# The two first tiles of the most frequent expert, routed from half of the tokens, prepared during attention

## The chip, the cores and the metric

One core of one Trainium2 chip runs the whole program. The metric is device time in microseconds of an execution. The engines are called as the profile calls them: PE (TensorE matmul; PEld its weight loads), DVE (VectorE), ACT (ScalarE), POOL (GpSimd), SP (SyncE, here a queue of DMA issues).

## What is computed

Three layers in float32, one after the other:

```
scores = q @ k^T / 8                     # 4 batches, 8 heads, 576 rows, 64 columns
keep scores >= row max - tau (0.02), softmax, @ v         -> x [2304, 512]
logits = x @ w_gate + modality_bias[modality_id]          # 8 experts
e = argmax(logits); gate = softmax(logits)[e]
out[row] = gate * (relu(x[row] @ w1[e]) @ w2[e])          # w1 512x1024, w2 1024x512
h = out @ w_in; g = h * sigmoid(1.702 h); result = g @ w_out   # w_in 512x2048
```

The modality bias (spread 0.5) dwarfs what x adds to the logits, so a row's expert is nearly its modality's. With the reference's inputs 2043 rows go to expert 1 and 261 to expert 4; of the 1152 rows of the first two batches, 1011 go to expert 1.

## The kernel before

The five engines run programs of their own that are tied by semaphores; each engine's order is the order in which its program is written.

**Attention.** Heads are handled in 16 pairs (one head of two batches), two pairs to a "quad"; pairs 0 to 7 belong to the first two batches. A pair has nine units of 128 query rows (`U = 9`), and a quad 18 steps. In step `i` PE transposes the probabilities of a unit five steps back and the q and k of the next pair (L1191, L1205), makes a unit's scores (L1225), and in steps u = 1 and 5 of a pair the product with v of the pair before (L1239), in u = 3 and 7 its turn to rows (`turn`, L1256 to L1264). DVE scales the scores with their row minimum (L760) and masks the unit of two steps earlier (L715); ACT exponentiates (L1038) and copies the transposed blocks out of PSUM (L1001, L1012); POOL makes the threshold (`thresh`, L626), splits the next pair's q and k in high and low parts (`split`, L576, L578) and swaps halves of k. `over_quads` writes quad 0 out, loops over quads 1 to 6, and writes quads 7 and 8 out (quad 8 has the last values and no scores).

Matrix products are exact to float32 by three passes: a high part in the reduced format, a low part (`x - high`), and high·high + low·high + high·low. Weights are loaded raw, copied to high by ACT (L1105), subtracted to low by DVE (L918).

**Routing.** After the last head DVE runs a chain of small operations, each waiting for the one before (`link`): logits of all 18 row tiles, the expert of each row, gates; PE counts rows per tile and expert (L1306, L1307); DVE works out each row's place in the list sorted by expert and two one-hot matrices (L838 to L844); PE multiplies them to the list of rows `table` (L1313); DVE writes the plan (tiles of 256 rows: `PL_AT` first place, `PL_END` the end of an expert's turn). The list is turned, stored in DRAM (`order_dram`), the gates too.

**Experts.** POOL gathers a tile's rows and gates by indirect DMA (L647, L649): the first from `table`, later ones after loading their indices from `order_dram` (L660). DVE scales, PE transposes (L1323), ACT and DVE split. Then `up` (L1332, 96 matmuls) and `down` (L1345, 96 matmuls). `over_turns` loops over the experts in use; `enter` splits the expert's weights, `body` does a tile and transposes the next one ahead. `tile_x` is a single buffer: the gather of tile t+1 waits for the transposes of tile t. SP loads an expert's eight weight pieces (L521, L527) once the previous expert's have been split. At the end comes the dense layer (L1378, L1395).

The first lines of `over_turns` and of PE's `body`:

```
with eng.Fori(0, turns) as turn:
    first = eng.value_load(plan_i[...PL_END + turn...])
    enter(turn, first)
    with eng.Fori(first, end) as tile:  body(turn, tile)
# PE's body:  up(tile); transpose_x(tile + 1); down(turn, tile)
```

## Time and profile before

| what | us |
|---|---|
| median of 3 runs (1042.2 to 1042.96) | 1042.36 |
| the profiled execution | 1042.66 |
| its span | 1041.0 |
| attention, to PE's last turn | 342.6 |
| from there to the first expert matmul | 40.1 |
| ten expert tiles | 382.8 to 624 |
| dense layer | to the end |

The span is what the profile sees between first and last instruction; 1.66 us lie around it. Busy: PE 976.8 us (94%), DVE 483.3 (46%), ACT 442.2 (42%), POOL 258.1 (25%). An engine that is busy most of the time in one stage can stand idle in the next, so the page's slices and the stretches are read stage by stage. All numbers of a timeline are microseconds from the span's start.

### The profile page before, as it was taken

The page shows a single profiled execution, that of the slowest core. Times are in us where ns is not written, and L with a number is a line of the kernel's source. Part 1 is how long each engine was busy: PE and PEld are TensorE (multiplying, and loading weights), DVE is VectorE, ACT ScalarE, POOL GpSimd, SP SyncE. Part 2 cuts the span into 40 slices and gives each one's busy share as a digit, 9 for nine tenths or more (in the row PEclk, how much of TensorE's full clock was granted, in tenths as well). Part 3 has the DMA queues.
Part 4 walks back from the last instruction along what each step waited for, and adds up shares of the span by engine and source line. Part 5 has one row for each costly group of instructions (what it writes and reads, how often), then busy time and mean ns, then how long its engine had stood idle before and what let it go on. Part 6 is the DMA issues. An engine that isn't in the chain of part 4 may idle for free.

```text
span 1041.0 us, 19901 instructions
## 1 busy us (share of the span) xinstructions
PE 976.8 (94%) x6496; PEld 870.6 (84%) x6497; DVE 483.3 (46%) x1076; ACT 442.2 (42%) x1004; POOL 258.1 (25%) x360
## 2 busy tenths in 40 slices
PE   5999999999998339999999999999999999999994
PEld 5777878778786239999999998989999999999994
DVE  6878778787787642212113335532322223222221
ACT  4777878787786041112113335432222222222221
POOL 5655656556552031112222100010010010100101
PEclk9999999999999659999999999999999999999998
DMA  3232222222211084111111443210000000000000
GB/s 81 49 64 63 51 63 58 54 64 63 60 31 24 12 278 146 40 40 40 50 50 41 149 144 112 61 52 11 31 30 0 30 30 30 31 0 0 31 1 31
DMA packets 103422, 57.18 MB, mean 55 GB/s; under 512 B 84917, under 2 KB 93659, under 8 KB 103387
## 3 DMA queue, kind: packets, MB, share of 16 engines
q1 hardware_dynamic: 92072, 40.15, 14.4%
q0 software_dynamic: 4224, 10.51, 3.2%
q10 hardware_dynamic: 7091, 6.08, 1.8%
q8 instruction: 18, 0.29, 0.1%
q14 instruction: 17, 0.14, 0.0%
HBM read 41.49 MB, written 15.22 MB: 54 GB/s over the span
## 4 chain that ended last, share of the span: by engine, by line
PE 89%; DVE 3%; issue 2%; POOL 1%; ACT 1%; DMA 1%; ACTq 0%; SPq 0%; POOLq 0%; DVEq 0%
PE s_ps L1395 19%; PE s_ps L1378 13%; PE s_ps L1332 11%; PE o_ps L1239 8%; PE pt_ps L1191 8%; PE s_ps L1225 8%; PE pt_ps L1378 6%; PE misc L1345 6%; PE o_ps L1345 6%; PE pt_ps L1205 3%; PE pt_ps L1323 1%; PE misc L1264 1%; PE misc L1256 1%; DVE probs L715 0%; DMA qk<-in_k_dram 0%
## 5 line engine op out<-in xcount | busy, mean ns | idle before, releaser
L978 DVE TENSOR_TENSOR g<-s_ps,sig 128x384 f32<-128x384 f32 x96 | 53.5, 558 | 279.1 <-ACT sig L1162 279.1
L1162 ACT ACTIVATE sig<-s_ps 128x384 f32<-128x384 f32 x96 | 47.2, 492 | 273.5 <-PE s_ps L1395 273.5
L760 DVE TENSOR_SCALAR_CACHE_REDUCE scores<-s_ps,taus 128x576 f32<-128x576 f32 x144 | 117.8, 818 | 61.9 <-PE s_ps L1225 39.8
L715 DVE SCALAR_TENSOR_TENSOR probs<-scores,thresh,probs 128x576 f32<-128x576 f32 x144 | 130.8, 909 | 0.0
L1191 PE MATMUL pt_ps<-ident,probs 128*128 128x128 f32 x720 | 126.7, 277 | 4.0 <-ACT pT L1001 2.7
L1395 PE MATMUL s_ps<-yT_high,w_in_high 128*128 (+1 forms) x384 | 129.5, 337 | 0.3 <-issue 0.2
L1395 PE MATMUL s_ps<-yT_high,w_in_low 128*128 (+1 forms) x384 | 129.5, 337 | 0.0
L1395 PE MATMUL s_ps<-yT_low,w_in_high 128*128 (+1 forms) x384 | 128.9, 336 | 0.0
L669 POOL DMA_INDIRECT out_dram<-out_sb,table x18 | 18.9, 1049 | 419.6 <-ACT out_sb L1137 416.0
L1038 ACT ACTIVATE probs<-scores,row_low 128x576 f32<-128x576 f32 x144 | 115.5, 802 | 10.9 <-DVE scores L760 9.2
L1191 PEld LDWEIGHTS pt_ps<-ident,probs 128*128 128x128 f32 x720 | 84.0, 140 | 26.6 <-issue 19.5
L626 POOL TENSOR_TENSOR thresh<-row_low,taus 128x1 f32<-128x1 f32 x144 | 74.0, 514 | 121.9 <-DVE scores L760 114.3
L1225 PE MATMUL s_ps<-qkT 128*128 128x288 f32 x320 | 101.7, 335 | 2.5 <-DVE k_swap L709 0.6
L1332 PE MATMUL s_ps<-xT_high,w_high 128*128 128x256 f32 x320 | 91.6, 286 | 8.8 <-DVE w_low L918 8.5
L1239 PE MATMUL o_ps<-pT,vv 128*64 128x320 f32 x640 | 93.2, 437 | 0.8 <-ACT pT L1001 0.8
L1332 PE MATMUL s_ps<-xT_low,w_high 128*128 128x256 f32 x320 | 91.2, 285 | 0.0
L1332 PE MATMUL s_ps<-xT_high,w_low 128*128 128x256 f32 x320 | 91.2, 285 | 0.0
L1225 PE MATMUL s_ps<-k_swap,qkT 128*128 128x288 f32 x320 | 89.2, 295 | 0.0
L1001 ACT COPY pT<-pt_ps 128x512 f32<-128x512 f32 x144 | 85.3, 592 | 8.8 <-PE pt_ps L1191 6.1
L908 DVE SCALAR_TENSOR_TENSOR hT_low<-s_ps,hT_high 128x512 fp32r<-128x512 f32 x40 | 27.6, 691 | 113.8 <-ACT hT_high L1082 113.8
L1395 PEld LDWEIGHTS s_ps<-yT_high,w_in_high 128*128 128x128 f32 x384 | 72.2, 188 | 5.1 <-issue 1.0
L1378 PE MATMUL s_ps<-w_out_high,g_low 128*128 128x512 f32 x192 | 76.2, 397 | 0.0
(209 smaller groups left out, 2205.5 us busy)
## 6 DMA issues: line engine op xcount, KB each, us to landing
w_raw<-in_moe_w_dram SPq DMA_DIRECT2D x16, 512.0 KB, 4.6
yT_dram<-tile_yT ACTq DMA_DIRECT2D x11, 512.0 KB, 2.9
x_dram<-xs SPq DMA_DIRECT2D x32, 128.0 KB, 2.0
w_in_raw<-in_moe_w_in_dram SPq DMA_DIRECT2D x4, 1024.0 KB, 6.2
w_out_raw<-in_moe_w_out_dram SPq DMA_DIRECT2D x16, 256.0 KB, 2.6
qk<-in_k_dram SPq DMA_DIRECT2D x30, 128.0 KB, 2.4
next_yT<-yT_dram SPq DMA_DIRECT2D x5, 768.0 KB, 4.5
qk<-in_q_dram SPq DMA_DIRECT2D x16, 128.0 KB, 2.2
```

Source lines behind the costliest of these rows:

```text
L626: pool.tensor_tensor(thresh[:, j, u:u + 1], row_low[:, j, u:u + 1], taus[:, 4:5], ALU.add).then_inc(thresh_ready, 1)
L715: dve.scalar_tensor_tensor(out=probs[:, i % PROB_SLOTS, 0:SEQ], in0=scores[:, i % SCORE_SLOTS], scalar=thresh[:, j, u:u + 1], in1=probs[:, ...
L760: dve.tensor_scalar(scores[:, i % SCORE_SLOTS].rearrange("p (c n) -> p c n", c=2), s_ps[i % 2][:, :, 0:HALF], taus[:, 3:4], None, ALU.mult ...
L1001: act.copy(pT[:, 0:TAIL, v * P:(v + 1) * P], pt_ps[:, 0:TAIL]).then_inc(keys_copied, 1)
L1038: act.activation(probs[:, k % PROB_SLOTS, 0:SEQ], scores[:, k % SCORE_SLOTS], ACT.Exp, bias=row_low[:, k // U, k % U:k % U + 1], scale=-1. ...
L1191: return pe.transpose(pt_ps[:, block], probs[:, k % PROB_SLOTS, block * P:(block + 1) * P], ident[:])
L1225: mm = pe.matmul(s_ps[i % 2][:, c, 0:HALF], qkT[j][:, 0, q_tile * P:(q_tile + 1) * P], keys[:, first:first + HALF], start=(at == 0), stop= ...
L1239: mm = pe.matmul(o_ps[lo:lo + DH, 0:UP], vv[j][:, side, block], pT[:, block, at:at + UP], start=(block == 0), stop=(block == TPB - 1))
L1332: mm = pe.matmul(hT_ps[f // 2][:, f % 2 * T:(f % 2 + 1) * T], w_part[:, a, f * P:(f + 1) * P], x_part[:, a], start=(a == 0 and part == 0), ...
L1345: mm = pe.matmul(yT_ps[d // 2][:, d % 2 * T:(d % 2 + 1) * T], w_part[:, f, d * P:(d + 1) * P], h_part[:, f], start=(f == 0 and part == 0), ...
L1378: mm = pe.matmul(mlp_y_ps[i], g_part[:, f % GT, at], w_part[:, f, :], start=(f == 0 and part == 0), stop=(f == FB2 - 1 and part == 2))
L1395: mm = pe.matmul(mlp_h_ps[f % 2], w_part[:, a, f * P:(f + 1) * P], y_part[:, bass.ds(c % 2 * DB + a, 1)].rearrange("p a b -> p (a b)"), st ...
```

## The change

- After pair 7 the first two batches are complete. `half_logits(0)`, `half_choice(0)`, `half_gates(0)` route their 1152 rows during quads 4 and 5; PE counts them in two small matmuls. `early_expert` picks the most frequent expert and limits its early rows to 512; `early_members` to `early_one_hots` make the list of its first 512 rows (two tiles), which PE writes in quad 6 (nine small matmuls).
- SP stores the first half's gates, loads the expert's w1 in quad 6 and w2 in quad 7. ACT and DVE split w1 in quad 7, one piece in each of four steps. POOL gathers tile 0 in steps 2 and 7 of quad 7. Part of `up(0)` stands between attention's last steps in quad 8, w2's split beside it.
- The full routing then runs beside the rest of `up(0)`, `down(0)`, `up(1)`. Experts are renumbered so that the early one is 0 and its early rows are the list's first 512; the plan counts tiles from 2 on (`EARLY`). Turn 0 is written out; `over_turns` runs from turn 1, which is the same expert again, its weights loaded and split a second time.
- Buffers are laid out anew so that the weights don't cover what attention still uses (w1_high over `xs0`, w2_raw over `qk`, and so on). Quads 4 to 7 are written out on all engines, SP's whole loop too. Gates are stored without being transposed, as single columns.

The core of the diff, first what holds for all engines:

```diff
+    EARLY = 2
+    EARLY_SLOTS = EARLY * T // P
...
-            with eng.Fori(1, QUADS - 1) as quad:
+            with eng.Fori(1, QPB) as quad:
                 step(quad)
-            for quad in range(QUADS - 1, last):
+            for quad in range(QPB, last):
                 step(quad)
```

On SP:

```diff
+            def early_part(quad, j):
+                if (quad, j) == (QUADS - 2, 0):
...
+                    store_gates(0)
+                if (quad, j) == (QUADS - 2, 1):
+                    sp.wait_ge(first_expert_ready, 1)
+                    load_w1(sp.value_load(first_expert_i[0:1], min_val=0, max_val=E - 1), 0)
+                if (quad, j) == (QUADS - 1, 1):
+                    sp.wait_ge(turned, UNITS)
+                    sp.wait_ge(order_stored, 16)
+                    load_w2(sp.value_load(first_expert_i[0:1], min_val=0, max_val=E - 1), 0)
...
+            store_gates(1)
+            sp.wait_ge(order_rows_ready, 1)
+            sp.dma_start(order_dram[0:N].rearrange("(t p) -> t p", p=P), order_rows[:]).then_inc(order_stored, 16)
             sp.wait_ge(plan_ready, 1)
```

On POOL:

```diff
+                    if isinstance(quad, int) and quad == QUADS - 1 and i in (2, 7):
+                        pool.wait_ge(x_stored[0], PAIRS // 2 * 4 * 16)
+                        pool.wait_ge(gate_stored, 4 * 16)
+                        pool.wait_ge(early_list_ready, 1)
+                        gather(early_list, 0, (2, 7).index(i), N // 2)
...
+                    if isinstance(quad, int) and quad == QUADS - 1 and i in (6, 10):
+                        pool.wait_ge(tile_x_loaded, (6, 10).index(i) * 32 + 32)
...
+            for tile in range(1, EARLY):
+                pool.wait_ge(xT_written, tile * 2)
                 for i in range(2):
+                    gather(early_list, tile * 2, i, N // 2)
```

On DVE:

```diff
+            def early_part(quad, i):
+                if (quad, i) == (QPB, 2):
+                    bias_of_rows()
+                if (quad, i) == (QPB, 11):
+                    half_logits(0)
+                if (quad, i) == (QPB, 14):
+                    half_choice(0)
+                    early_hot()
+                if (quad, i) == (QPB + 1, 0):
+                    half_gates(0)
+                if (quad, i) == (QPB + 1, 2):
+                    early_expert()
+                if (quad, i) == (QPB + 1, 5):
+                    early_members()
+                if (quad, i) == (QPB + 1, 9):
+                    early_places()
+                if (quad, i) == (QPB + 1, 12):
+                    early_split()
+                if (quad, i) == (QPB + 1, 15):
+                    early_one_hots()
+                if (quad, i) == (QPB + 2, 4):
+                    early_list_part()
+                if quad == QUADS - 1 and i in (2, 6, 11, 15):
+                    a = (2, 6, 11, 15).index(i)
+                    split_w_low(w1_low, w1_raw, w1_high, w1_high_ready, w1_low_ready, a, a)
+                if (quad, i) == (QUADS - 1, 13):
+                    scale_x(0)
+                if quad == QUADS and i in (6, 7):
+                    split_w_low(w2_low, w2_raw, w2_high, w2_high_ready, w2_low_ready, i - 6, i - 6)
+                if (quad, i) == (QUADS, 2):
+                    xT_low_part(0, first_xT_ps)
```

On ACT:

```diff
+            def early_part(quad, i):
+                if (quad, i) == (QPB, 16):
+                    half_expos(0)
+                if quad == QUADS - 1 and i in (1, 5, 10, 14):
...
+                    split_w_high(w1_high, w1_raw, w1_loaded, w1_high_ready, 0, (1, 5, 10, 14).index(i))
+                if (quad, i) == (QUADS, 2):
+                    xT_high_part(0, first_xT_ps)
+                if quad == QUADS and i in (6, 7):
...
+                        split_w_high(w2_high, w2_raw, w2_loaded, w2_high_ready, 0, a)
```

On PE (the first piece is in `transpose`):

```diff
+                if extra in ("ranks", "totals"):
+                    pe.wait_ge(hot_ready, 1)
+                    pe.matmul(extra_ps[:, 0:U * E], (before if extra == "ranks" else ones)[:],
+                              hot[:, 0:U].rearrange("p t e -> p (t e)"), start=True, stop=True)
+                if extra == "list":
...
+            def early_part(quad, i):
+                if (quad, i) == (QUADS, 0):
+                    pe.wait_ge(low_ready, UNITS - 1)
+                    transpose_x(0, first_xT_ps)
+                if (quad, i) == (QUADS, 4):
...
+                if quad == QUADS and i in (4, 5, 6):
+                    up_block(FIRST_UP[i - 4])
...
+            for f in FIRST_UP[3:6]:
+                up_block(f)
...
+            for f in FIRST_UP[6:]:
+                up_block(f)
...
+            transpose_x(1)
+            pe.wait_ge(w2_low_ready, DB)
+            for d in range(2):
+                down_block(0, d)
+            pe.wait_ge(hT_low_ready, 4)
             pe.wait_ge(one_hot_ready, 2)
             for n in range(RT):
                 mm = pe.matmul(table_ps, row_hot[:, n], slot_tok[:, n], start=(n == 0), stop=(n == RT - 1))
             mm.then_inc(table_written, 1)
+            pe.wait_ge(ranks_read, 1)
+            for d in range(2, DB):
+                down_block(0, d)
             pe.wait_ge(order_ready, 1)
             pe.transpose(order_ps, order_sq[:], ident[:]).then_inc(order_turned, 1)
...
+            pe.wait_ge(table_ready, 1)
+            pe.wait_ge(xT_low_ready, 4)
+            for f in range(FB1):
+                if f == 2:
+                    pe.wait_ge(order_rows_ready, 1)
+                up_block(f)
+            transpose_x(2)
+            down(1)
             pe.wait_ge(plan_ready, 1)
-            transpose_x(0)
             over_turns(pe, enter, body)
```

(An `up_block` is 12 matmuls, a `down_block` 24.)

**Where rows move on POOL.** POOL's program in steps 1 to 7 of quad 7, attention's pair 14, before (in square brackets the semaphores waited for; `qk_parts` is what PE transposes in step 5):

```order
L586 COPY k_swap_51<-qkT_49 64x576 [waits turned_copied,thresh_ready]
L588 COPY k_swap_51<-qkT_49 64x576 [waits k_swapped]
L626 TENSOR_TENSOR thresh<-row_low,taus 128x1 [waits probs_ready,low_ready,k_swapped]
L576 CAST qk_parts<-qk 128x8x64 [waits turned,qk_b_loaded]
L578 TENSOR_TENSOR qk_parts<-qk,qk_parts 128x8x64 [waits parts_ready]
L626 TENSOR_TENSOR thresh<-row_low,taus 128x1 [waits probs_ready,low_ready] x4
L586 COPY k_swap_52<-qkT_50 64x576 [waits turned_copied,thresh_ready]
L588 COPY k_swap_52<-qkT_50 64x576 [waits k_swapped]
```

and with the change:

```order
L654 COPY k_swap_55<-qkT_53 64x576 [waits turned_copied,thresh_ready]
L656 COPY k_swap_55<-qkT_53 64x576 [waits k_swapped]
L687 DMA tile_x<-x_dram,early_list 128x512 [waits gate_stored,early_list_ready,x_stored0,k_swapped]
L689 DMA tile_gate<-gate_dram,early_list 128x1
L705 TENSOR_TENSOR thresh<-row_low,taus 128x1 [waits probs_ready,low_ready]
L644 CAST qk_parts<-qk 128x8x64 [waits turned,qk_b_loaded]
L646 TENSOR_TENSOR qk_parts<-qk,qk_parts 128x8x64 [waits parts_ready]
L705 TENSOR_TENSOR thresh<-row_low,taus 128x1 [waits probs_ready,low_ready] x4
L654 COPY k_swap_56<-qkT_54 64x576 [waits turned_copied,thresh_ready,tile_x_loaded]
L656 COPY k_swap_56<-qkT_54 64x576 [waits k_swapped]
L687 DMA tile_x<-x_dram,early_list 128x512 [waits gate_stored,early_list_ready,x_stored0,k_swapped]
L689 DMA tile_gate<-gate_dram,early_list 128x1
```

The two indirect DMAs of tile 0's first half stand ahead of step 2's threshold and of the split, and a second two ahead of step 7's threshold.

**Where rows move on DVE.** DVE's program with the change, from the one-hot `hot` of all rows (after the last head) to the scaling of tile 2; between the pieces stand the small operations of routing that are also there before:

```order
L1015 TENSOR_TENSOR hot<-expert_less,choice 128x144 [waits route]
...
L921 TENSOR_TENSOR w_low<-w_raw,w_high 128x1024 [waits w2_high_ready] x2
L927 TENSOR_SCALAR tile_x<-tile_x,tile_gate 128x512 [waits tile_x_loaded] x2
L1022 COPY in_tile<-misc 128x144 [waits tiles_counted]
...
L940 SCALAR_TENSOR_TENSOR hT_low<-s_ps,hT_high 128x512 [waits hT_high_ready,route]
L940 SCALAR_TENSOR_TENSOR hT_low<-s_ps,hT_high 128x512 [waits hT_high_ready] x3
L1034 TENSOR_TENSOR place_e<-place_e,rows_first 128x144 [waits ranks_read]
...
L1048 TENSOR_TENSOR slot_hot<-place_slot,iota_row 128x324 [waits x_stored1,split_ready]
L1052 TENSOR_TENSOR slot_tok<-slot_hot,token_id 128x324 [waits split_ready]
L1054 TENSOR_TENSOR row_hot<-place_row,iota_row 128x2304
L933 TENSOR_TENSOR xT_low<-pt_ps,xT_high 128x512 [waits xT_high_ready] x2
...
L1109 CAST order_rows<-s_ps 18x128 [waits order_turned]
L940 SCALAR_TENSOR_TENSOR hT_low<-s_ps,hT_high 128x512 [waits hT_high_ready] x3
L927 TENSOR_SCALAR tile_x<-tile_x,tile_gate 128x512 [waits tile_x_loaded] x2
```

The chain of routing, which stood alone, now has the low parts of w2 and of tiles 0 and 1 in between, and `order_rows` ahead of tile 1's `hT_low`.

## Rows read from the trace of the kernel before

**Rows 1.** Stretches: us, busy time of each engine (instructions), granted clock, DMA share, GB/s

```profile
182.00:208.00 26.00, 25.89 (x202) 20.47 (x199) 20.48 (x53) 19.93 (x50) 15.28 (x22) 1.00 0.25 55
312.00:338.00 26.00, 23.34 (x169) 16.48 (x167) 19.73 (x56) 16.79 (x38) 6.58 (x11) 1.00 0.10 24
```

**Rows 2.** PE timeline: start us, us, line, operation, out<-in [idle before <-releaser]

```profile
341.92 0.70 PE L1264 MATMUL misc<-turn_and_gate,oT 128*128 128x144 f32 x4
...
347.76 0.84 PE L1306 MATMUL misc<-hot,before 128*128 128x144 f32 x2 [5.13 <-DVE hot L807]
...
356.38 4.01 PE L1313 MATMUL o_ps<-slot_tok,row_hot 128*128 128x18 f32 x18 [7.08 <-DVE row_hot L844]
...
372.32 1.94 PE L1323 MATMUL pt_ps<-ident,tile_x 128*128 128x128 f32 x8 [9.12 <-DVE tile_x L895]
...
382.78 0.57 PE L1332 MATMUL s_ps<-xT_high,w_high 128*128 128x256 f32 x1 [8.51 <-DVE w_low L918]
```

**Rows 3.** DVE timeline, routing and the first gathered tile

```profile
343.23 2.21 DVE L800 TENSOR_REDUCE logits<-xs 128x144 f32<-128x1152 f32 x1
...
353.77 2.55 DVE L844 TENSOR_TENSOR row_hot<-place_row,iota_row 128x2304 fp32r<-128x2304 f32 x1
...
362.41 0.18 DVE L884 CAST plan_i<-plan 1x64 int32<-1x64 f32 x1
...
371.30 0.88 DVE L895 TENSOR_SCALAR tile_x<-tile_x,tile_gate 128x512 f32<-128x512 f32 x2 [7.77 <-DMA tile_gate<-gate_dram,table]
```

**Rows 4.** Chain that ended last, expert tiles: start us, us, what

```profile
382.78 13.35 PE s_ps L1332 x96
...
408.50 11.52 PE s_ps L1332 x96
...
432.40 11.52 PE s_ps L1332 x96
...
576.11 11.77 PE s_ps L1332 x96
```

**Rows 5.** Stretches in the gap and after it; PEclk is the column after POOL

```profile
343.00:346.00 3.00, 0.00 (x0) 0.00 (x0) 2.90 (x4) 0.00 (x0) 0.00 (x0) 0.90 0.26 56
386.00:387.00 1.00, 1.00 (x9) 1.00 (x9) 1.00 (x2) 0.41 (x1) 0.05 (x1) 0.82 0.62 226
```

**Rows 6.** Groups by form: busy us, mean ns of one | idle before

```profile
L918 DVE TENSOR_TENSOR w_low<-w_raw,w_high 128x1024 fp32r<-128x1024 f32 x16 | 18.4, 1221 | 8.5 <-ACT w_high L1105 8.5
...
L908 DVE SCALAR_TENSOR_TENSOR hT_low<-s_ps,hT_high 128x512 fp32r<-128x512 f32 x40 | 27.6, 691 | 113.8 <-ACT hT_high L1082 113.8
```

**Rows 7.** DVE and PE timelines, around bias_of_rows in pair 15

```profile
315.76 0.67 DVE L735 TENSOR_SCALAR mod_zero<-mod_one 128x18 f32<-128x18 f32 x1
...
317.98 0.81 DVE L760 TENSOR_SCALAR_CACHE_REDUCE scores<-s_ps,taus 128x576 f32<-128x576 f32 x1
...
318.95 0.37 PE L1225 MATMUL s_ps<-qkT 128*128 128x288 f32 x1 [0.17 <-DVE scores L760]
```

**Rows 8.** POOL and PE timelines, pair 14 of attention

```profile
297.82 0.64 POOL L626 TENSOR_TENSOR thresh<-row_low,taus 128x1 f32<-128x1 f32 x1 [0.66 <-PE pt_ps L1191]
...
299.09 1.29 POOL L578 TENSOR_TENSOR qk_parts<-qk,qk_parts 128x512 fp32r<-128x512 f32 x1
...
302.13 0.19 POOL L626 TENSOR_TENSOR thresh<-row_low,taus 128x1 f32<-128x1 f32 x1 [1.09 <-DVE scores L760]
...
300.81 0.38 PE L1205 MATMUL pt_ps<-ident,qk_parts 128*128 128x128 f32 x2
```

**Rows 9.** POOL timeline, index load and gather of the second tile

```profile
376.18 0.99 POOL L647 DMA_INDIRECT tile_x<-x_dram,tile_index  x1 [3.35 <-DMA tile_index<-order_dram]
...
380.10 1.97 POOL L649 DMA_INDIRECT tile_gate<-gate_dram,tile_index  x1 [0.30 <-issue]
...
385.30 0.75 POOL L660 DMA_DIRECT2D tile_index<-order_dram  x1 [3.23 <-DMA tile_gate<-gate_dram,tile_index]
```

**Rows 10.** SP's issues of an expert's w1: start us, us until all four are issued

```profile
364.50 6.56 SPq L521 DMA_DIRECT2D w_raw<-in_moe_w_dram  x4
```

More of the change, by code:

```diff
@@ L656, in _ @@
             tiles = tiles_of(pool)
-            with pool.Fori(1, tiles + 1) as tile:
-                at = place_of(pool, tile + 1)
+            with pool.Fori(EARLY, tiles + 1) as tile:
+                at = place_of(pool, tile)
                 wait_apart(pool, tile_x_loaded, tile * 64)
@@ L1337, in down @@
-            def down(turn, tile):
-                wait_apart(pe, w2_low_ready, (turn + 1) * DB + 1)
-                wait(pe, tile_yT_copied, tile * 2 + 2)
-                for d in range(DB):
-                    for f in range(FB1):
-                        if d == 0 and f % 2 == 0:
-                            wait(pe, hT_low_ready, tile * 4 + f // 2 + 1)
-                        for part, (w_part, h_part) in enumerate(((w2_high, hT_high), (w2_high, hT_low), (w2_low, hT_high))):
-                            mm = pe.matmul(yT_ps[d // 2][:, d % 2 * T:(d % 2 + 1) * T], w_part[:, f, d * P:(d + 1) * P],
-                                           h_part[:, f], start=(f == 0 and part == 0), stop=(f == FB1 - 1 and part == 2))
-                    if d % 2 == 1:
-                        mm.then_inc(tile_yT_written, 1)
```

620 lines of the change are left out of this document (399 added, 221 removed).

## The prediction

> **What bounds the kernel now.** I read the stretches first, then each engine's timeline where PE is not busy. Through attention PE is the bound: in a stretch of 26 us it is busy 25.89 us, DVE 20.48, ACT 19.93, POOL 15.28; in the stretch that reaches into attention's tail PE has already 2.66 us without work [rows 1]. The PE timeline shows the hole behind it: the last turn of attention starts at 341.92 and ends at 342.6, the first expert matmul starts at 382.78, and between them stand only a few small products, each behind a wait [rows 2]. So 40.1 us pass in which the critical work is DVE's chain of routing (343.23 to 362.6 [rows 3]), the first gather (DVE has tile 0 at 371.30 after 7.77 us of waiting for it [rows 3]) and the split of w1 (8.51 us of waiting on DVE [rows 2]). From then on PE is the bound again: a tile costs 23.9 us (408.50 to 432.40 [rows 4]) and the first one 25.7 (382.78 to 408.50), for the clock had halved: it averages 0.90 from 343 to 346, which puts the fall (from 2.4 to 1.2 GHz) at about 345.4, 2.8 us after PE's last work, and it comes back during 386 to 387, 3.4 us after the first expert matmul [rows 5].
>
> **The change, part by part.** I keep before's times as the clock and add attention's extra length, s, at the end.
>
> *In attention (s).* PE gets two counts of 72 columns: one of 144 columns takes 0.84 us at half clock [rows 2], so half the columns at full clock a quarter, 0.4 us for both, and nine list products, 4.01/18 = 0.22 us each at half clock, 0.11 at full, 1.0 us [rows 2]: 1.4 us on PE, which has no slack. ACT copies these three results between its copies of the transposed blocks: 0 if covered, 3 x 0.18 (a small operation [rows 3]) if not; I take 0.5, since PE waits for those copies each step.
>
> DVE gets some 45 small operations of 0.2 to 0.3 us, a one-hot of half the size of row_hot (1.3 us of 2.55 [rows 3]), four low parts of w1 (4 x 1.22 [rows 6]) and scaling (0.88 [rows 3]): 16 us in quads 4 to 7, which have 160 us and of them 21% idle, 34 us [rows 1]. What an insertion costs PE is shown by one that is there now: bias_of_rows holds DVE from 315.6 to 317.98, 2.4 us, and PE then waits 0.17 us [rows 7]. No inserted piece is longer than 1.7 us, and most stand in steps next to a values product. I take 0.3 us for all; the other end is in the rivals. ACT's four copies of w1 (taken as long as DVE's low parts, 1.22) stand where PE does a values product: nothing. What covers them is that product; without it they would cost 4.9.
>
> POOL gets the first gather pair ahead of step 2's threshold and split in pair 14. In before that threshold starts at 297.82, the split ends at 300.38 and PE takes its result at 300.81: slack 0.43 us [rows 8]. Two indirect DMAs cost 2x + 0.3 us with x between 0.95 and 1.97 (0.99, and 1.97 beside a busy DVE [rows 9]). With x = 1.2, near the many and not the one, PE waits 2.7 - 0.4 = 2.3 us. The second pair (step 7) delays only a threshold that DVE needs some 3 us later: nothing at this x. SP puts w1 and w2 (6.56 us to issue four pieces [rows 10]) ahead of loads of v and q that are issued over 10 us ahead of their use: nothing; were that lead gone, each would cost up to 6.6. That quads 4 to 7 are written out costs nothing I can see: pairs 14 and 15 were already. **s = 1.4 + 0.5 + 0.3 + 2.3 = 4.5 us.**
>
> *End of attention.* Quad 8 takes up eight transposes (0.9) and three blocks of up(0), 12 matmuls x 0.12 = 1.44 each (11.52/96 [rows 4]), 5.2 together, and in exchange fills 2.7 us of waits (2.66 by 338 [rows 1]): PE's last turn ends at 345.1 instead of 342.6.
>
> *Routing beside PE.* PE: five blocks (7.2) and the counts (two of 0.84 at half clock, 0.65 with their start) to 352.95, transposes of tile 1 to 353.8. DVE until then: the second half's logits to hot, 3.5 us (half of 2.21 and eleven small ones), gates 0.65, two low parts of w2 2.2 (their high parts are done at 344), scaling 0.9, and then, before hT_low, six operations of routing, 1.9: at 354.8 it starts hT_low (0.69 each [rows 6]), so PE starts down(0) at 355.55: **1.75 us waited.** Two of its blocks end at 361.3. DVE goes on: four hT_low, eight small operations, the two one-hots and row_hot (2.55) to 362.95: **1.65 us waited.** The table takes 2.0 us at full clock, two more blocks 5.76, the order's transpose 0.25: 370.95. up(1) needs nothing late and ends at 382.5. Both waits are under the 2.8 us after which the clock fell.
>
> *Tile 2 is late next.* DVE reads the turned order after the low part of tile 1 (1.4), 21 plan operations (4.6), and 15 more (3.2): 372.7. Its store (no row shows its landing; a later load's 3.35 us of waiting [rows 9] bounds it above, an issue of 0.3 below, and I take 2.4, nearer the load), POOL's loads of the plan (0.5), the index load (0.75 + 3.35 = 4.1 [rows 9]) and the gather (from 376.18 to 385.30 is 9.1 us [rows 9]; the first one 7.6 to DVE's start at 371.30) follow one another: 388.3 with 8.6 for the gather; scaled at 389.2. **PE waits 6.7 us** (3 to 10, if each link is at its short or long end). The clock falls again, so the eight transposes take 1.94 us [rows 2] and not 0.87, and down(1) starts slow: 11.5 + 0.75. The turn change that follows costs 0.3 us of issue, as between the tiles at 576.11 [rows 4]; the second split of the same expert (eight pieces x 1.22 = 9.8 us on DVE [rows 6]) lies beside down(1) and up(2). up(2) starts at 389.2 + 1.95 + 12.25 + 0.35 = 403.75; in before it starts at 432.40 [rows 4]. That is 28.65 us earlier, less s = 4.5: **24.1 us.** Eight tiles and the dense layer remain as they were. Against the profiled execution, 1042.66 - 24.1 = 1018.5; that execution stands 0.3 us over the median, so I leave 1018.5 as it is. A measurement of this kernel tells 0.2% (2 us) from no change.
>
> **The rivals.**
> - *Tile 2 is nearly in time.* All links short: the stall is 2 us, below 2.8, and the clock stays, which gives back 4.7 + 1.8: 1012. For: at tile 2's gather DVE does little that could slow it. Against: four links must all be at their short end, 7.6 us and less for the gather alone.
> - *Attention doesn't absorb the insertions.* For: DVE's idle is in pieces of 0.2 to 1.2 us, so half of the 16 us may fall on PE: +8, 1026.5. Against: bias_of_rows [rows 7].
> - *POOL's indirect DMAs are held up by DVE.* The same threshold takes 0.64 us or 0.19 [rows 8], depending on what DVE does, and one gather step took 1.97 for 0.99 [rows 9]. If an indirect DMA can run only in DVE's 21% idle [rows 1], x = 1.05/0.21 = 5 us, the two pairs hold PE for (2x - 0.1) + (2x - 2.9) = 4x - 3 = 17 us instead of 2.3: 1033. The Trainium skill's page "SBUF — State Buffer" (SBUF: two separate sides, and the part on the bandwidth-pool intuition) says that DVE and GpSimd share a port pair by an exclusive lock and that descriptors made by GpSimd starve meanwhile, 620 ns becoming 3100. By that factor of five on the 1.0 us here the estimate is the same 17 us and 1033; the trace bears out a factor of two once and none in three others.
> - *Slower than before*: the same mechanism, further. Without any gather stall the change gives 26.4 us; 4x - 3 exceeds that from x = 7.4 us. At 8 us each: 1045. Only steady DVE work with no gap would do it, and attention has gaps.
> - *No early tile gained.* Had the first half fewer than 512 rows of the expert, the rest would need one tile more, 23.9 us, and the time would be 1042.5. The inputs give 1011.
>
> **How the numbers follow.** Forecast 0.58; tile 2 in time 0.12; attention longer 0.17; gathers held 0.09; slower 0.03; no tile 0.01. The range 1012 to 1028 takes in the forecast with its own bounds (stall 3 to 10, s 2.5 to 9: 1013 to 1025), the first rival's value and the second's, and leaves out the last three and some tails. Faster: 0.95, all but the last two; same 0.02; slower 0.03.
>
> **What would show it.** Right: PE's last turn near 349.6, with a wait of 2 to 3 us in pair 14 on qk_parts; up blocks before that turn; waits of some 1.7 us before down(0) and before the table's products; one of 5 to 8 us on tile_x after up(1), with the clock at half behind it; up(2) near 408. Wrong: PE's busy time per stretch in quads 4 to 6 clearly under 25.8, indirect DMAs on POOL of over 2 us each, or tile 2 scaled before up(1) ends.

## The result, and the profile after

| | kernel before | changed kernel |
|---|---|---|
| median of 4 runs each, same chip | 1042.66 us | 1032.01 us (1030.36 to 1032.43) |
| ratio | | 0.9892, 95% interval 0.9881 to 0.9904 |
| forecast | | 1018.5 (1012 to 1028) |
| profiled execution, and its span | 1042.66, 1041.0 | 1031.82, 1030.2 us |
| up(2) starts (third tile) | 432.40 [rows 4] | 421.49 us; forecast 408.3 |
| last product with v in attention starts | 338.22 | 351.15 us |
| PE's last turn starts | 341.92 [rows 2] | 357.14 us; forecast 348.9 (its end 349.6) |

The change is faster by 10.7 us, and 24.1 were forecast. From up(2) on the two traces run alike, a tile every 23.9 us as in [rows 4], so the missing microseconds, 13.2 between these traces, lie ahead of 421.5 us. Two numbers place them. The last turn starts 8.2 us later than forecast: attention is longer than I priced it. From its start to up(2) it takes 64.35 us where the forecast has 59.35: 5.0 us more behind attention.

The first view is that of what PE waits for between 160 and 425 us in the changed kernel (engine, what was written, who released it: us in total, times, the longest):
```profile
PE pt_ps L1512 <- DVE tile_x L927: 8.0, 1, 8.0
PE pt_ps L1426 <- POOL qk_parts L646: 5.6, 5, 3.2
PE pt_ps L1412 <- ACT pT L1197: 1.5, 5, 0.7
PE o_ps L1602 <- DVE hT_low L940: 1.5, 1, 1.5
PE s_ps L1629 <- DVE row_hot L1054: 1.0, 1, 1.0
PE s_ps L1455 <- POOL k_swap L656: 1.0, 2, 0.5
PE s_ps L1455 <- DVE scores L990: 0.8, 1, 0.8
```
Every wait that was forecast is there: tile 2 (6.7 said), POOL's split (2.3 said, 3.2 for the one in pair 14), hT_low (1.75 said), row_hot (1.65 said). But the waits inside attention that it lists add up to 8.9 us, 5.5 more than the 3.4 of the kernel before, and attention is 12.9 us longer. Over half of that is in no wait that this view names. It shows in how much PE does in a stretch. First the kernel before, then the changed one, from 182 to 262 us (us; busy us and instructions of PE, PEld, DVE, ACT, POOL; granted clock, DMA share, GB/s):
```profile
182.00:262.00 80.00, 79.60 (x614) 63.97 (x612) 63.64 (x161) 63.64 (x160) 46.37 (x68) 1.00 0.27 60
```
```profile
182.00:262.00 80.00, 75.58 (x567) 58.38 (x565) 72.87 (x185) 58.97 (x147) 42.78 (x61) 1.00 0.25 53
```
In the same 80 us PE does 47 matmuls fewer of 614, and DVE goes from 63.6 to 72.9 us: of the 16.4 us that were its idle time, 7.1 are left.

**Where in attention.** The products with v, one in each of the steps 1, 5, 10 and 14 of a quad, mark equal places of the loop. Some of their starts in the changed kernel, from (4, 1) on, in PE's timeline (start, us, instruction):
```profile
172.12 2.91 PE L1469 MATMUL o_ps<-pT,vv 128*64 128x320 f32 x20
182.25 2.91 PE L1469 MATMUL o_ps<-pT,vv 128*64 128x320 f32 x20
...
300.29 2.91 PE L1469 MATMUL o_ps<-pT,vv 128*64 128x320 f32 x20
313.80 3.49 PE L1469 MATMUL o_ps<-pT,vv 128*64 128x320 f32 x20
```
In the kernel before these starts are 9.3 and 10.7 us apart in turn, through all of quads 4 to 6. In the changed kernel, with the DVE operations inserted in each interval (their us from DVE's timeline):

| from step | 4, 1 | 4, 5 | 4, 10 | 4, 14 | 5, 1 | 5, 5 | 5, 10 | 5, 14 | 6, 1 | 6, 5 to 7, 1 | 7, 1 |
|---|---|---|---|---|---|---|---|---|---|---|---|
| inserted | bias 2.4 | 0 | logits 2.0 | choice, gates 1.8 | expert 1.9 | members, places 2.6 | split 2.2 | one-hots 2.1 | list 0.2 | 0 | gather on POOL, w1 |
| before | 9.3 | 10.7 | 9.3 | 10.7 | 9.3 | 10.7 | 9.3 | 10.7 | 9.3 | 30.7 | 9.3 |
| after | 10.1 | 10.7 | 10.2 | 11.2 | 10.7 | 11.6 | 11.0 | 11.9 | 10.2 | 30.7 | 13.5 |

The additions, some 15 us of them on DVE, made quads 4 to 6 longer by 8.0 us (172.12 to 300.29 against 172.31 to 292.47). The interval of the first gather is longer by 4.2, and the rest up to the last product with v by 0.9: 13.1, and 12.9 with a start that is 0.2 earlier. PE's own additions in quads 4 to 6, the two counts and the nine list products, are 1.7 us busy; the list products stand in the interval from (6, 1), where DVE does almost nothing extra.

**How a small operation gets long.** DVE's timeline has in the piece of quad 5 that divides the places:
```profile
244.15 0.17 DVE L898 TENSOR_SCALAR place_row_i<-place_i 128x9 int32<-128x9 int32 x1
244.36 1.13 DVE L899 TENSOR_SCALAR place_slot_i<-place_i 128x9 int32<-128x9 int32 x1
```
and POOL's timeline of the same moment:
```profile
244.17 1.29 POOL L646 TENSOR_TENSOR qk_parts<-qk,qk_parts 128x512 fp32r<-128x512 f32 x1
```
The second operation of DVE, 0.17 us of work like the first, ends with POOL's at 245.5. This suggests that an idle microsecond of DVE is no free one while POOL has work; the runs below with pads test it.

**The gather of pair 14.** POOL's timeline, and PE's first product behind it:
```profile
306.38 1.34 POOL L687 DMA_INDIRECT tile_x<-x_dram,early_list  x1 [0.29 <-POOL k_swap L656]
308.01 1.41 POOL L689 DMA_INDIRECT tile_gate<-gate_dram,early_list  x1 [0.30 <-issue]
309.49 0.19 POOL L705 TENSOR_TENSOR thresh<-row_low,taus 128x1 f32<-128x1 f32 x1
309.61 0.61 POOL L644 CAST qk_parts<-qk 128x512 fp32r<-128x512 f32 x1
310.30 1.65 POOL L646 TENSOR_TENSOR qk_parts<-qk,qk_parts 128x512 fp32r<-128x512 f32 x1
312.01 0.69 PE L1426 MATMUL pt_ps<-ident,qk_parts 128*128 128x128 f32 x2 [3.21 <-POOL qk_parts L646]
```
The row of PE is from its own timeline. Two indirect DMAs took 3.0 us with the gap, for 2.7 forecast; the split behind them took 1.65 for 1.29, and PE waited 3.2. The granted clock (the column after POOL's) fell behind that wait, to 1.2 GHz:
```profile
312.00:314.00 2.00, 1.99 (x9) 1.71 (x11) 0.09 (x1) 1.05 (x3) 0.25 (x2) 0.50 0.00 0
```

**Behind attention.** The stretches of the changed kernel around tile 0's down blocks (columns as above):
```profile
378.00:382.00 4.00, 4.00 (x20) 4.00 (x21) 3.45 (x19) 0.00 (x0) 0.00 (x0) 0.50 0.00 0
384.00:386.00 2.00, 2.00 (x19) 2.00 (x18) 0.52 (x4) 0.00 (x0) 0.00 (x0) 1.00 0.00 0
```
The clock stood at half (1.2 GHz) from 378 to 382, which the forecast excluded, and was back at 2.4 GHz from 384. And the chain of work that ended last, from the copy of the order to up(2) (start, us, what):
```profile
375.48 3.10 PE s_ps L1629 x18
378.57 7.99 PE misc L1602 x48
386.70 0.29 DVE order_rows L1109
387.01 1.28 DMA order_dram<-order_rows
...
391.39 4.50 DMA tile_index<-order_dram
...
400.69 4.47 DMA tile_gate<-gate_dram,tile_index
405.18 0.89 DVE tile_x L927 x2
406.12 1.97 PE pt_ps L1512 x8
408.09 6.91 PE o_ps L1602 x48
415.00 5.75 PE misc L1602 x48
```
Two blocks of down cost 7.99 and later, at the full clock, 5.75.

### The profile page after: what moved, and what is told of

It is laid out like the page before. It is cut to its first block, busy times and chain, and to the rows that moved or that the text cites. A ratio compares the mean times of both kernels' runs of the same rounds, so it can differ in the third digit from the quotient of the medians.

```text
span 1030.2 us, 18968 instructions
## 1 busy us (share of the span) xinstructions
PE 982.1 (95%) x6508; PEld 873.9 (85%) x6509; DVE 507.6 (49%) x1134; ACT 449.5 (44%) x1013; POOL 259.9 (25%) x358
## 4 chain that ended last, share of the span: by engine, by line
PE 79%; DVE 7%; issue 6%; POOL 3%; ACT 2%; DMA 1%; POOLq 0%; DVEq 0%; SPq 0%; ACTq 0%
PE s_ps L1679 19%; PE s_ps L1662 13%; PE s_ps L1520 9%; PE pt_ps L1662 6%; PE o_ps L1469 6%; PE misc L1602 6%; PE o_ps L1602 5%; PE pt_ps L1412 5%; PE s_ps L1455 5%; DVE probs L792 3%; PE pt_ps L1426 2%; DVE scores L990 1%; PE pt_ps L1512 1%; POOL qk_parts L646 1%; ACT probs L1282 1%
## 5 line engine op out<-in xcount | busy, mean ns | idle before, releaser
L792 DVE SCALAR_TENSOR_TENSOR probs<-scores,thresh,probs 128x576 f32<-128x576 f32 x144 | 136.0, 946 | 0.0
L1662 PE MATMUL s_ps<-w_out_low,g_high 128*128 128x512 f32 x192 | 75.8, 395 | 0.0
```

Of the source, the lines that this page charges most:

```text
L792: dve.scalar_tensor_tensor(out=probs[:, i % PROB_SLOTS, 0:SEQ], in0=scores[:, i % SCORE_SLOTS], scalar=thresh[:, j, u:u + 1], in1=probs[:, ...
L1662: mm = pe.matmul(mlp_y_ps[i], g_part[:, f % GT, at], w_part[:, f, :], start=(f == 0 and part == 0), stop=(f == FB2 - 1 and part == 2))
```

## The experiments

All are edits of the changed kernel unless said otherwise; the medians of "before" beside them were 1042.4 to 1043.5. The 95% intervals of the ratios are about 0.0012 wide to each side, so two kernels less than some 2.5 us apart are not told apart by their times alone. A pad is a small operation that is added only to take time. The theory at the start: DVE was taken for an engine with 21% to spare, and it has less. The rivals: the written-out quads, the breaks as such, PE's and ACT's additions; and for the gather, that it costs wherever it stands.

### Where the first gather stands
```
-                    if isinstance(quad, int) and quad == QUADS - 1 and i in (2, 7):
+                    if isinstance(quad, int) and quad == QUADS - 1 and i in (4, 7):
...
-                        gather(early_list, 0, (2, 7).index(i), N // 2)
+                        gather(early_list, 0, (4, 7).index(i), N // 2)
```


> The changed kernel (1032.0 us) with the first gather pair of quad 7 issued in step 4, behind POOL's split of qk_parts in step 2, and not ahead of it. In the changed kernel PE waits 3.2 us for that split at 308.8 us, and its granted clock then falls to 0.83 in the stretch 310 to 320, which I price at 1.5 to 2 us. Theory: both belong to the gather's place alone: 1027, PE's wait for qk_parts in pair 14 under 0.5 us, and the clock 1.00 in every stretch from 300 to 320. Rival: two indirect DMAs delay POOL's next threshold wherever they stand, so the wait only moves: 1031 to 1032.

Measured: 1026.72 us (1025.51 to 1026.93), ratio to before 0.9843 (0.983 to 0.9855). POOL splits first and gathers then:
```profile
307.23 1.29 POOL L646 TENSOR_TENSOR qk_parts<-qk,qk_parts 128x512 fp32r<-128x512 f32 x1
...
309.36 1.15 POOL L687 DMA_INDIRECT tile_x<-x_dram,early_list  x1 [0.18 <-DVE probs L792]
```
The long interval is 9.4 us and not 13.5, PE does not wait for the split, the clock is 1.00 from 308 to 316, and the last product with v starts 4.4 us earlier; the other microsecond came behind attention, where the clock was at half for less long (two down blocks 7.21 us, not 7.99). The same two DMAs cost about 4.1 us of attention in one place and nothing that shows two steps later. The rival falls.

### More DVE work in the same places
```
+                if (quad, i) in ((QPB, 11), (QPB, 14), (QPB + 1, 0), (QPB + 1, 2), (QPB + 1, 5),
+                                 (QPB + 1, 9), (QPB + 1, 12), (QPB + 1, 15)):
+                    for _ in range(6):
+                        link(dve.tensor_tensor(pad[:], bias_all[:, 0:U], bias_all[:, 0:U], ALU.add))
```


> The changed kernel with six more small DVE operations (128x72, 0.26 us each with their wait, written to a scratch tile) at each of eight places in quads 4 and 5 where it has a piece of routing: 48 x 0.26 = 12.5 us of DVE. Theory of a full DVE: in the 80 us from 182 to 262 of the kernel before, DVE waited for PE only 9.7 us in 8 times; the changed kernel put 14.7 us there and 1.3 us of waiting is left, so every further microsecond lies on the path: 1032.0 + 12 = 1044. Rival A, the cost is that of a break and not of its length: eight longer breaks, 1034 or less. Rival B, the prediction's step (insertions are absorbed): 1032.3.

Measured: 1048.08 us, 16.1 more for 12.5. Steps (4, 1) to (6, 1) took 102.5 us (87.3 in the changed kernel), and PE now waits for DVE itself, from 200 to 280 us:
```profile
PE s_ps L1459 <- DVE scores L994: 8.2, 4, 3.1
```
Absorption is out, and so is a price per break. Once DVE is full a further microsecond costs 1.2 here (15.2 for 12.5). Two things can make it more than 1, and were not told apart: some pads were stretched (up to 1.61 us), and the clock was lower in places (granted 0.83 from 225 to 235 and from 255 to 265).

### Only the writing out
The kernel before, with nothing but this on every engine (on SP the whole loop is written out, as in the changed kernel):
```
-            with eng.Fori(1, QUADS - 1) as quad:
+            with eng.Fori(1, QPB) as quad:
                 step(quad)
-            for quad in range(QUADS - 1, last):
+            for quad in range(QPB, last):
```


> The kernel before (1042.7 us) with quads 4 to 7 written out on every engine instead of run by a loop, and nothing else. Theory of a full DVE: writing out costs nothing, 1042.7 within 1 us. Rival: part of attention's extra length in the changed kernel comes from the written-out code (fetching instructions, SP's longer program): 1045 or more.

Measured: 1042.72 us (11 runs), ratio 0.9996 (0.9987 to 1.0005). Writing out costs nothing that can be measured.

### The same routing in twelve pieces
```
+            SLOTS = [(q, i) for q in (QPB, QPB + 1, QPB + 2) for i in (2, 6, 11, 15)]
...
+                if (quad, i) in SLOTS:
+                    next(pieces)
```


> The changed kernel with the same DVE operations of early routing cut into twelve pieces of at most 1.4 us and placed in quads 4, 5 and 6 only ahead of the score copy of steps 2, 6, 11 and 15, where DVE waits 1.2 us for PE behind a values product; ranks, totals and the list product move to later steps to suit. Theory of a full DVE: 12 such waits of 1.2 us take 14.5 us, nearly all of the 14.7 us: of the 6.4 us that quads 4 and 5 are longer, about 1 us is left: 1026.5 us. Rival A, each break has a price of its own: twelve breaks for ten, 1032 to 1034. Rival B, the length comes from PE's and ACT's additions and not from DVE: 1032.

Measured: 1029.53 us (1028.89 to 1030.89): 2.5 us back, not 5.5. Quads 4 to 6 are longer by 5.8 and not 8.0, a bit in nearly every interval that has a piece. PE and ACT do the same additional work, in later steps, so what came back came from where the additions stand; but the 1.2 us in which DVE waits for PE behind a product with v were not free. POOL works just there. In the kernel before, DVE's timeline has these two waits for PE:
```profile
186.11 0.82 DVE L760 TENSOR_SCALAR_CACHE_REDUCE scores<-s_ps,taus 128x576 f32<-128x576 f32 x1 [1.17 <-PE s_ps L1225]
...
196.87 0.82 DVE L760 TENSOR_SCALAR_CACHE_REDUCE scores<-s_ps,taus 128x576 f32<-128x576 f32 x1 [1.29 <-PE s_ps L1225]
```
and POOL's, of the same times:
```profile
184.93 0.71 POOL L576 CAST qk_parts<-qk 128x640 fp32r<-128x640 f32 x1
185.72 1.56 POOL L578 TENSOR_TENSOR qk_parts<-qk,qk_parts 128x640 fp32r<-128x640 f32 x1
...
195.94 0.66 POOL L586 CAST k_swap<-qkT 64x576 fp32r<-64x576 f32 x1 [0.33 <-POOL thresh L626]
```
A split fills the first, and the swap, of which a second half follows, most of the second.

### Pads in those steps, and beside them
Four pads of 0.26 us at four steps of quad 6, `(2, 6, 11, 15)` in one kernel and `(0, 4, 9, 13)` in the other.

> The changed kernel with four small DVE operations on a scratch tile in SBUF (128x72, 0.26 us each) at each of four places in quad 6, ahead of the score copy of steps 2, 6, 11 and 15: 4.2 us of DVE in the places where it waits 1.2 us for PE behind a values product. Read from the starts of the values products in quad 6 (10.7, 9.3 and 10.7 us apart without additions). Theory of slots (DVE alone is full): free, quad 6 longer by under 0.5 us. Theory of a pair, DVE and POOL: an operation of DVE that reads only SBUF and POOL's operations hold each other up (L899 took 1.13 us for 0.17, L899 of the kernel in slots 1.48 for 0.23), and steps 2 and 6 are where POOL splits and swaps: single pads of 0.6 to 1.5 us, quad 6 longer by about 2 us.

> The same four times four pads of 0.26 us in quad 6, at steps 0, 4, 9 and 13, where POOL has neither split nor swap to do. Theory of slots: DVE is late there and has to catch up in the next wait for PE, so about as free as in the slots or up to 1 us dearer. Theory of a pair: all pads at 0.26 us and quad 6 longer by less than with the pads in steps 2, 6, 11 and 15, under 1 us.

Measured: 1038.04 us in the slots (4 runs) and 1034.99 beside (2 runs); the forty microseconds of quad 6 were 3.9 and 1.5 us longer, both more than expected. The groups of DVE by line from 255 to 310 us, in the slots:
```profile
L793 DVE SCALAR_TENSOR_TENSOR probs<-scores,thresh,probs 128x576 f32<-128x576 f32 x23 | 21.6, 938 | 0.0
...
L949 DVE TENSOR_TENSOR pad<-bias_all 128x72 f32<-128x72 f32 x16 | 9.0, 565 | 0.4
```
and beside them:
```profile
L793 DVE SCALAR_TENSOR_TENSOR probs<-scores,thresh,probs 128x576 f32<-128x576 f32 x24 | 25.5, 1061 | 0.0
...
L949 DVE TENSOR_TENSOR pad<-bias_all 128x72 f32<-128x72 f32 x16 | 3.7, 230 | 0.4
```
The same 16 operations take 9.0 us or 3.7, by what POOL does at the time. The theory of slots falls, that of the pair holds. But the pads beside POOL's work save 5.3 us and quad 6 only 2.4: the mask (`probs`), which also reads only SBUF, now takes 1.061 us on average for 0.938. What no longer meets POOL as a pad meets it, in part, as a mask.

### What holds them: the source
The same pads at steps 2, 6, 11 and 15 behind the wait for the scores, with two sources:
```
+                                link(dve.tensor_scalar(pad[:], s_ps[i % 2][:, 0, 0:72], 1.0, None, ALU.mult))
```
and
```
+                                link(dve.tensor_scalar(pad[:], bias_all[:, 0:U].rearrange("p t e -> p (t e)"), 1.0, None, ALU.mult))
```


> The changed kernel with four pads at each of steps 2, 6, 11 and 15 of quad 6 again, but behind the wait for the scores, and each a DVE operation that reads 128x72 from PSUM (the scores' bank) and writes the scratch tile. If what POOL's work holds up is an operation of DVE that reads only SBUF (a port that the two share), these pads take under 0.3 us each, with none over 0.5; if POOL's work holds DVE whatever it reads, they take 0.5 to 0.6 us on average as the pads of the fifth kernel did.

> The partner of the run before it: the same four times four pads at the same places behind the wait for the scores, each reading 128x72 from SBUF. Theory of a shared port: mean over 0.4 us, some 0.7 to 1.5 us long, and attention longer by 1 us or more than with the pads that read PSUM. Rival: the same durations and the same length.

Measured: 1034.32 and 1037.43 us, one execution each. Durations in ns (min/median/max), first the pads that read PSUM, then those that read SBUF:
```profile
L989 DVE TENSOR_SCALAR pad<-s_ps x16: 231/232/233, 264.6 to 296.4; 128x72 f32<-128x72 f32 x16
```
```profile
L989 DVE TENSOR_SCALAR pad<-bias_all x16: 198/199/1494, 265.1 to 299.9; 128x72 f32<-128x72 f32 x16
```
A pad from PSUM never takes over 0.233 us; one from SBUF takes 0.198 or is held, up to 1.49, and quad 6 is longer by 2.2 and 5.1 us. In both kernels POOL splits or swaps beside all four groups of pads. This is what the Trainium skill says in "SBUF — State Buffer" (SBUF: two separate sides, and Who interferes with whom): the port pair of DVE and GpSimd is a lock held for a whole instruction, and a DVE operation outside the fast modes, in which it uses both pairs of ports, does not need it if at most one input is in SBUF. The traces here agree: 16 of 16 pads from PSUM went through. The pad from SBUF has a single SBUF input too, so by that rule it must be in a fast mode to be held; its 0.198 us for 0.231 fits that, and no run here changes the mode alone.

### The routing beside POOL's work
`SLOTS` with steps `(0, 4, 9, 13)`, and the products of ranks and totals at steps 1 and 2 of quad 5.

> The changed kernel (1032.0) with its 14.7 us of early routing on DVE in the twelve pieces of the kernel in slots (1029.5), but placed at steps 0, 4, 9 and 13 of quads 4 to 6, where POOL has no split and no swap. Theory of a pair: 4.2 us of pads cost 3.9 us of quad 6 in the slots and 1.6 beside POOL's work (0.4 per us), so quads 4 to 6 are longer by about 5 us and not 8.3 (as placed in the changed kernel) or 8 (in slots, into quad 7): 1028. Theory of DVE's length alone: the same as in slots, 1029.5 or more.

Measured: 1032.61 us (1030.92 to 1033.59): nothing gained. But one interval of quad 5 was 13.8 us for 10.7, with a wait of PE of 1.7 us for hot, which DVE writes one step ahead of the product: my own placement made it.

### The order of work behind attention
DVE splits w2's last parts ahead of the last row scaling, reads the table first; PE turns the order one block sooner:
```
+                if (quad, i) == (QUADS, 8):
+                    for a in range(2, DB):
+                        split_w_low(w2_low, w2_raw, w2_high, w2_high_ready, w2_low_ready, a, a)
...
-            for d in range(2, DB):
-                down_block(0, d)
+            down_block(0, 2)
             pe.wait_ge(order_ready, 1)
             pe.transpose(order_ps, order_sq[:], ident[:]).then_inc(order_turned, 1)
+            down_block(0, 3)
```


> The changed kernel (1032.0) with the work behind attention in another order: DVE splits the last two parts of w2 ahead of the last row scaling (it waits 4.1 us for PE there), reads the table before it works at the plan, PE turns the order behind the third of tile 0's down blocks and not the fourth, and DVE copies the turned order in the middle of the plan. Theory: PE's waits of 1.5 us for hT_low and 1.0 us for row_hot go, the clock (granted 0.50 from 378 to 382) does not fall in down(0), and the order is stored 6.6 us earlier (387.0 to 380.4), so up(1) starts 5.7 us earlier and the wait for tile_x stays at 7 to 8 us: up(2) at 415.5 and not 421.5, 1026. Rival: the chain of store, index load and gather is held by something else (SP's queue, the weights' loads), and only the first part is gained: 1030.

Measured: 1029.99 us (1029.49 to 1030.47): 2.0 us, not 6, as the rival had it, and the intervals of this kernel and the changed one overlap. The first half came: no wait for hT_low, 0.7 us for row_hot, and the clock stays in this execution.
```profile
378.00:382.00 4.00, 4.00 (x36) 4.00 (x35) 3.46 (x17) 0.00 (x0) 0.00 (x0) 1.00 0.00 0
```
The order was ready at 381.6 and not 386.7, in spite of an attention that was 1.2 us longer in this execution. But the index load started only at 387.97, and the two transfers were as slow:
```profile
387.97 4.42 DMA tile_index<-order_dram
...
397.18 5.29 DMA tile_gate<-gate_dram,tile_index
```
So the rest turned into a longer wait for tile 2 (9.4 us). POOL waits for the whole plan (ready at 385.0) as well as for the order. That the shorter wait is what kept the clock is not shown: the last three kernels below have the same single wait of 0.7 us, and there it fell to 0.50 all the same, from 369 to 375 us in the last but one.

### The second turn's loads
```
+                sp.wait_ge(tile_x_loaded, (EARLY + 1) * 64)
                 load_w1(expert, turn)
```


> The changed kernel with SP's loads of the second turn's weights held back until tile 2 has been gathered. In the changed kernel those loads are issued from 389.1 to 404.7 us, beside the index load (5.5 us from issue to its use, DMA share 0.80) and the gather (8.3 us). Theory of contention: with the loads away the index load takes 4.1 us as in the kernel before, and the wait for tile_x falls from 8.0 to 6 us: 1030, as w1's parts (loaded by 412, split by 417) are still in time for up(2) at 419. Rival: no contention, or the later loads are waited for: 1032 or more.

Measured: 1028.65 us (1026.93 to 1029.34), 3.4 us less. The chain, as above:
```profile
391.89 2.46 DMA tile_index<-order_dram
...
399.13 2.67 DMA tile_gate<-gate_dram,tile_index
```
2.0 us are saved at the index and 1.8 at the last gather; the wait for tile 2 is 4.1 us and not 8.0. The weights, loaded 13 us later, are still in time.

### All together
The gather, the placement, the order of work, six plan operations ahead of the table, and the loads:

> The changed kernel with all edits together: the first gather behind POOL's split (measured alone: -5.3 us), the pieces at steps 0, 4, 9 and 13 (expected -4), the order of work behind attention of the seventh kernel (-2.0) with six plan operations put into DVE's wait for the table (-1), and the second turn's loads behind tile 2's gather (-3.4). If they add up: 1032.0 - 15.7 = 1016. Rival: they overlap, since an earlier order only lengthens the wait for tile 2 and a later gather meets other work: 1020 or more.

Measured: 1019.84 us (1018.58 to 1020.78), 3.8 above the sum of 1016; the 13.4 us interval with the wait for hot is there too. The next kernel moves the two products to steps 3 and 4, and the last one lets POOL go on with its part of the plan:
```
+            dve.tensor_copy(plan_i[:, PL_TILES:], plan[:, PL_TILES:]).then_inc(tiles_planned, 1)
...
-            pool.wait_ge(plan_ready, 1)
+            pool.wait_ge(tiles_planned, 1)
```


> The kernel with all edits, with the products for ranks and totals two steps later (steps 3 and 4 of quad 5, not 1 and 2). In the two kernels that place routing beside POOL's work the interval with these products took 13.8 and 13.4 us for 10.7, with a wait of PE of 1.7 us for hot, which DVE writes only one step ahead. Theory: this wait, made by my own placement, is what hid the gain of that placement: attention 3 us shorter, 1019.8 - 3 = 1017, and that interval at 11.2 us. Rival: the interval is long for the pieces in it, and the time stays at 1019 to 1020.

> The kernel of the run before it, with the part of the plan that POOL reads (the number of tiles and their places) converted on its own ahead of the other 15 plan operations, and POOL waiting for that part alone. In the kernel with all edits the order is stored at 377.2 us, but POOL begins to load the plan's values only at 380.5, behind plan_ready, and PE waits 3.5 us for tile 2. Theory: index load and gather start 2 us earlier and that wait falls to 1.5 us: 2 us below the run before it. Rival: the store's landing is what is late, and nothing is gained.

Measured: 1016.09 us (1015.57 to 1017.94), the interval at 11.0, and 1015.14 us (1014.01 to 1015.4), ratio to before 0.9733 (0.972 to 0.9747). PE's longest wait from 160 to 420 us in the last one:
```profile
PE pt_ps L1514 <- DVE tile_x L944: 2.1, 1, 2.1
```
It fell from 3.0 to 2.1, half of what I had expected, and the chain now goes through the store itself (1.29 us) and not through the plan. The index load does start 1.9 us sooner behind the turned order, but it took 3.69 us for 2.80. The last two kernels are 0.95 us apart; their runs do not overlap, but the intervals of their ratios do, so the times alone do not show a gain for certain. The last one beats the kernel before by 27.7 us and the changed one by 16.9.

## Why the prediction was wrong

Point by point, against its own steps:

- **What bounds the kernel, and the gain without s**: right in its parts. The first turn's work is hidden, two tiles run in the hole, and tile 2 is late next, where it was said to be.
- **"What an insertion costs PE is shown by one that is there now"** (0.17 us for 2.4): this step failed, and it cost 5.8 of the 8.2 us that the last turn was late. The row was real [rows 7] but came from pair 15, where POOL has no split left and PE fewer transposes. The same operations in quad 4 cost 0.8 us. I had also read the 21% of idle DVE time [rows 1] as free, and it is not: from 182 to 262 us of the kernel before, DVE waits for PE 9.7 us in 8 pieces of 1.2, and the other 6.0 us are waits of at most 0.2 us for its own last operation, POOL's threshold and ACT; and POOL is at work in the long ones. In the changed kernel 1.3 of the 9.7 us are left. For PE, ACT and DVE's insertions I said 2.2 us together, and 8.0 were measured. PE's additions are 1.7 us busy, for 1.4 said, so nearly all of the miss is DVE's term of 0.3. The work was undersized as well: 16 us for all, where some 15 stood in quads 4 to 6 and w1's low parts and the scaling come to nearly 6 more. The rival "attention doesn't absorb the insertions", at +8, had the place, and its number on top of the forecast (1026.5) was still 5.5 short; it had 0.17, and deserved the larger part.
- **POOL's gather, 2.3 us**: right in place and mechanism, mis-sized by 1.9 (4.2). x came to 1.34 and 1.41, not 1.2; the split took 1.65 for 1.29; and behind the wait of 3.2 us the clock was at 0.50 from 312 to 314. The rival of x = 5 falls: the 4 early gathers of tile_x took 0.95 to 1.34 us each. The factor of five of the Trainium skill's page "SBUF — State Buffer" (the part on the bandwidth-pool intuition), which would give the same x, did not appear: the most was 1.41 for 0.95.
- **Writing out, SP's loads, w1's copies: nothing**: right for the first by its own run. In the kernel with the gather moved, quad 7 with its w1 parts was within 1 us of before. The loads of w1 and w2 beside attention were not tried alone.
- **"Both waits are under the 2.8 us after which the clock fell"**: failed. The waits were 1.5 and 1.0 us, smaller than said, and yet the clock was at 0.61 from 376 to 378 and 0.50 to 382. So a single wait against the 2.8 us of one earlier fall was the wrong test. The fall cost 2.2 us in two down blocks (7.99 for 5.76) and 1 us in the table's products (3.10 for 2.16 in the kernel where it stayed). What sets it off stays open: it came behind a single wait of 0.7 us in three kernels and did not in a fourth. The order was turned 28.7 us behind the end of the last turn and not 25.85.
- **Tile 2's chain, 6.7 us of wait**: 8.0, and near by luck, for its links missed in both directions. From the turned order to the end of its store it took 1.9 us (DVE 1.75 and 2.4 said), POOL's reading of the plan 2.4 (0.5 said), the index load 6.1 with its issues (4.1 said), the gather 8.3 (8.6 said). The last two were costed from rows that stand beside a load of weights (DMA share 0.77 to 0.91 from 368 to 384 us in the kernel before); here SP issues the next turn's weights from 389.1 on, beside them again. Those loads are 3.9 us of the wait by the run that holds them back, and 3.4 of the time, and no term of the prediction names them.
- **Down(1) and the turn change**: 15.4 us from tile 2's transposes to up(2), 14.55 said; the down blocks took 12.66 for 12.25, the change of turn 0.7 for 0.3.

The sum of what was missed: 5.8 for the insertions, 1.9 for POOL and 0.7 in the rest of attention, less 0.2 of start, are the 8.2 ahead of the last turn; 2.9 to the end of up(1), 1.3 more of waiting for tile 2 and 0.8 behind it are the 5.0 after.

Small slips of the prediction's working, none of which decides anything: by its own way of reading, the clock came back 3.6 us after the first expert matmul and not 3.4; DVE's times 354.8 and 372.7 are each 0.55 us more than the terms named before them; and with both bounds at their long end the forecast would be 1026 and not 1025.

What stays open: how the 5.2 us by which quads 4 to 6 are still longer in the best kernel divide into DVE's length and the lock. With pieces of the same size the steps beside POOL's work and those with it differ by only 0.6 us (5.2 and 5.8), far less than the pads said. The masks of all of attention show part of the reason. First the kernel before, then the best one (by line: busy us, mean ns):
```profile
L715 DVE SCALAR_TENSOR_TENSOR probs<-scores,thresh,probs 128x576 f32<-128x576 f32 x144 | 130.8, 909 | 0.0
```
```profile
L794 DVE SCALAR_TENSOR_TENSOR probs<-scores,thresh,probs 128x576 f32<-128x576 f32 x144 | 141.1, 981 | 0.0
```
In the kernel with the pieces in POOL's steps they are 134.4 us, so moving the pieces out of these steps let masks in: 6.7 us more of them. The collisions moved in part. Most of what the placements gave may then come from cutting into small pieces over three quads, but no run separates the two.

## What to carry to other kernels

Price an insertion by a step that is loaded like its own, on every engine that shares something with it; the share of idle time says nothing until it is split into what waits for the bound engine and what is a gap between dependent operations. Mark equal places of a loop (here the products with v) and compare their distances in two traces: it finds within a tenth of a microsecond what the list of waits spreads over several lines or does not name. And when a transfer becomes the critical link, look at what the other queues start at that moment: a load that is not needed for 20 us can wait for it.

## What was unexpected of the hardware

DVE operations of 0.17 to 0.23 us that read only SBUF took up to 1.6 us beside a POOL operation (226/432/1611 ns min/median/max for the pads in steps 2, 6, 11 and 15), while one that reads PSUM stayed at 231 to 233 ns. Indirect DMAs were hardly slower beside a busy DVE: 0.95 to 1.41 us for the early ones. The 4 MB of a turn's weights, loaded on SP's queue, made a small index load and the last step of a gather beside them 4.5 us each; in the four kernels that hold the weights back they took 2.5 to 3.7 and 2.5 to 2.8. The granted clock fell behind waits of which none was over 1.5 us, and in three kernels behind a single one of 0.7 us ahead of the table's 18 small products.
